# Placing VectorE's inversion of the softmax sums before or behind the row maximum in a fused attention and feed-forward kernel

## What is computed

```python
def _attn_ref(q, k, v) -> np.ndarray:
    B, H, S, D = q.shape
    factor = 2
    scale = 1.0 / np.sqrt(D)
    q_pool = q.reshape(B, H, S // factor, factor, D).mean(axis=3)
    scores = scale * np.matmul(q_pool, k.transpose(0, 1, 3, 2))
    scores = scores - np.max(scores, axis=-1, keepdims=True)
    attn = np.exp(scores)
    attn = attn / (np.sum(attn, axis=-1, keepdims=True) + 1e-09)
    return np.matmul(attn, v).astype(np.float32)
...
    h = x @ w_in
    g = np.maximum(h, 0.0) + alpha * np.minimum(h, 0.0)
    return (g @ w_out).astype(np.float32)
```

## Time and profile before

| | |
|---|---|
| median of 3 runs | 898.81 us (898.24 to 899.74) |
| the profiled execution | 899.53 us, span 897.7 us |
| TensorE matmul | 846.3 us, 94% of the span |
| TensorE weight load | 653.1 us, 73% (beside the matmuls) |
| VectorE | 517.0 us, 58% |
| ScalarE | 424.8 us, 47% |
| GpSimd | 406.7 us, 45% |
| granted TensorE clock, mean | 0.998 |
| attention | to about 480 us |

### The profile page before, as it was taken

The page is one execution under the profiler, slowest core; times in us unless marked ns, Lnnn a source line. Parts: engine busy times, 40 slices in busy tenths (PEclk is TensorE's granted clock), DMA queues, the critical chain, the costliest instruction groups (busy, mean ns, idle before and its releaser), DMA issues. The chain is left out here.

```text
span 897.7 us, 20876 instructions
## 1 busy us (share of the span) xinstructions
PE 846.3 (94%) x6897; PEld 653.1 (73%) x6897; DVE 517.0 (58%) x792; ACT 424.8 (47%) x939; POOL 406.7 (45%) x320
## 2 busy tenths in 40 slices
PE   2899999999999999999999999999999999999996
PEld 1566666666665656666566899998999998999995
DVE  3677677776777777777774443445444445444442
ACT  2566666666666666766663222224222224222222
POOL 3656557555575556755532223223323323332330
PEclk9999999999999999999999999999999999999999
DMA  7344454434544445434321221223222122312211
GB/s 166 110 121 101 122 144 123 119 94 121 143 124 99 111 125 143 114 99 106 84 81 62 60 70 58 61 67 99 90 60 69 58 71 85 104 58 68 61 36 70
DMA packets 37518, 84.37 MB, mean 94 GB/s; under 512 B 6512, under 2 KB 10608, under 8 KB 37488
## 3 DMA queue, kind: packets, MB, share of 16 engines
q1 hardware_dynamic: 35088, 79.27, 33.0%
q10 hardware_dynamic: 2400, 4.72, 1.5%
HBM read 79.18 MB, written 4.79 MB: 94 GB/s over the span
## 5 line engine op out<-in xcount | busy, mean ns | idle before, releaser
L769 PE MATMUL slot_ps<-kq 128*128 128x384 f32 x1152 | 218.0, 337 | 1.4 <-PEq L766 1.4
L769 PEld LDWEIGHTS slot_ps<-kq 128*128 128x128 f32 x1152 | 204.3, 188 | 11.2 <-issue 3.3
L550 DVE TENSOR_REDUCE neg_max<-s_ps 128x1 f32<-128x1152 f32 x144 | 194.8, 1353 | 20.6 <-DVEq L549 19.9
L785 PE MATMUL s_ps<-kq 128*128 128x512 f32 x720 | 182.4, 394 | 2.1 <-PEq L782 2.1
L690 PE MATMUL s_ps<-kq 64*128 64x512 f32 x960 | 151.5, 424 | 8.9 <-PEq L701 4.4
L453 ACT ACTIVATE e_sb<-s_ps,neg_max 128x1024 f32<-128x1024 f32 x144 | 159.8, 1110 | 0.0
L717 PE MATMUL pv_ps<-pt,v_f 128*64 128x256 f32 (+1 forms) x1152 | 155.1, 412 | 0.2 <-PEq L736 0.2
L785 PEld LDWEIGHTS s_ps<-kq 128*128 128x128 f32 x720 | 133.4, 188 | 26.6 <-issue 3.7
L405 POOL TENSOR_TENSOR kq<-wi_raw,kq 128x512 fp32r<-128x512 f32 x48 | 64.6, 1347 | 152.4 <-POOLq L404 152.4
L413 POOL TENSOR_TENSOR kq<-wo_raw,kq 128x512 fp32r<-128x512 f32 x48 | 64.5, 1343 | 139.6 <-POOLq L412 139.6
L717 PEld LDWEIGHTS pv_ps<-pt,v_f 128*64 128x64 f32 x1152 | 76.7, 136 | 68.7 <-issue 25.5
(11 more groups left out here) (49 smaller groups left out, 699.5 us busy)
## 6 DMA issues: line engine op xcount, KB each, us to landing
q_raw<-in_q SPq DMA_DIRECT2D x62, 320.0 KB, 4.3
k_raw<-in_k SPq DMA_DIRECT2D x62, 288.0 KB, 4.2
wi_raw<-in_w_in SPq DMA_DIRECT2D x48, 256.0 KB, 2.6
wo_raw<-in_w_out SPq DMA_DIRECT2D x48, 256.0 KB, 2.6
v_f<-in_v SPq DMA_DIRECT2D x32, 288.0 KB, 3.7
out<-pt ACTq DMA_DIRECT2D x6, 768.0 KB, 3.9
inv_bc<-sums SPq DMA_DIRECT2D x32, 80.0 KB, 2.6
inv_bc<-sums SPq DMA_DIRECT2D x32, 64.0 KB, 3.7
```

What stands on the lines that cost most here:

```text
L550: nc.vector.tensor_reduce(out=neg_max[:, b:b + 1], in_=s_ps[:, S_AT[b]:S_AT[b] + NKEY], op=ALU.max, axis=AX_X, negate=True).then_inc(max_r ...
L769: ins = nc.tensor.matmul(slot_ps[h][:, 0:TOK], w[i][:, d * P:(d + 1) * P], x[h][:, d * TOK:(d + 1) * TOK], start=(d == 0 and w is wi_hi an ...
L785: ins = nc.tensor.matmul(y_ps[h][t], g[h][:, t * P:(t + 1) * P], w[i], start=(first == 0 and j == 0), stop=(last == 1 and j == 2))
```

## The change

`INVERT` becomes two tables, one for each g, and the call moves from between the two copies to the end of VectorE's step, behind the row maximum. The inversion of group 1 that stood in steps t = 0 of g = 0 goes to t = 1. The last one, with no pair behind it, is called where `left` is negative, which is step 144 alone. The order on the other engines is unchanged, and the same instructions are issued.

```diff
--- before.py
+++ after.py
@@ -56,7 +56,9 @@
     PRODUCT = [{1: (1, 1, (0, 1, 2)), 3: (1, 1, (3, 4, 5)), 5: (1, 1, (6, 7, 8)), 7: (0, 0, (0, 1, 2, 3, 4))},
                {0: (0, 1, (5, 6, 7, 8)), 2: (1, 1, (0, 1, 2, 3, 4)), 4: (1, 1, (5, 6, 7, 8)),
                 6: (0, 0, (0, 1, 2, 3, 4)), 8: (0, 0, (5, 6, 7, 8))}]
-    INVERT = {5: 0, 0: 1}
+
+
+    INVERT = [{5: 0, 1: 1}, {5: 0, 0: 1}]
 
     SCALE = [{0: 0, 6: 1}, {1: 0, 5: 1}]
     FIRST = 7
@@ -583,8 +585,6 @@
                     dve.wait_ge(tr_ready[1], 1).then_inc(tr_ready[1], -1)
                     nc.vector.tensor_copy(pt_half((s - 1) % TILES, 1),
                                           half_columns(slot_ps[1][:, :])).then_inc(slot_free[1], 1)
-                if t in INVERT and (INVERT[t] == 0 or pair is not None):
-                    invert(INVERT[t])
                 if s % 2 == 0:
 
                     dve.wait_ge(bank2_ready, 1).then_inc(bank2_ready, -1)
@@ -595,6 +595,10 @@
 
                         dve.wait_ge(even_cut_done, 1).then_inc(even_cut_done, -1)
                     row_max(s + 2)
+                if t in INVERT[g] and (INVERT[g][t] == 0 or pair is not None):
+                    invert(INVERT[g][t])
+                elif left < 0:
+                    invert(1)
 
             def unit(f, h):
                 dve.wait_ge(h_ready, 1).then_inc(h_ready, -1)
```

## The result

The changed kernel takes 914.77 us (median of four runs, 911.15 to 916.04) against 899.27 for the kernel before (median of four): a ratio of 1.0167, 95% interval 1.0136 to 1.0198. The forecast was 903.9. The direction was right, the size was a third of what came. The profiled execution took 914.39, 14.9 more than that of before, and its span is 912.6.

The account below looks back on a forecast made before the run. TensorE, busy 94% of the span, was taken to bound the kernel. Seven repeats +2.2, the start +1.6 and the clock +1.3 sum to +5.1 on the median 898.81: 903.9 us, range 901.0 to 906.5.

Parts of the forecast that it names:

- The path: Inversion leaves the row maximum's chain and delays the next step's scale and `slot1` copy, so TensorE's pause moves.
- step 60 at +0.25: After the inversion of t = 5, g = 0: later scale and copy lengthen step 60 by 0.25 us.
- step 56 at -0.15: Group 1's inversion moved to t = 1, g = 0: row maximum comes sooner, step 56 0.15 us shorter.
- step 64 at +0.20: After the inversion of step 63: later scale and copy lengthen step 64 by 0.20 us.
- nothing lost at t = 5, g = 1 and at the end: Steps 14, 32, ... 140 and the last inversion (step 144): later inversions cost TensorE nothing, 0.
- no scale waiting for late sums after step 18: Later sums still reach their scale in time; the opposing rival, chance 0.06, gave 910.9.
- the chain at the start: Step 5's later store delays head 4's queries, GpSimd, head 5's keys and step 14's scale: +1.6 us.
- the fall of the clock behind it: Step 14's pause grows to about 3.5 us, the clock drops to half in steps 15 and 16: +1.3 us.
- The order terms: Seven repeats of 0.27, 0.20 and -0.15 us from the new order on VectorE: +2.2 us.
- t = 0, g = 1: Steps 27, 45, ... 135, shown for 63: inversion behind the row maximum delays scale and copy, +0.20 us each.
- The list of rivals: Five: clock stays up 902.6 (0.23); start hidden 901.0 (0.09); waits go 892.1 (0.07); nothing changes 898.8 (0.08); late sums 910.9 (0.06).
- The clock term: +1.3 us for half clock after step 14's pause; the rival that it stays up had 0.23, 902.6.

Follow-up runs that it names:

- the one-input run: Changed kernel with an inversion's two half-sums added by a reduction over one tensor, the 1e-9 left out; 905.79 us, ratio 1.0077.
- run 5: Kernel before with only the inversion of t = 5, g = 0 moved behind the row maximum in loop and tail, two inputs; 922.97 us, ratio 1.0255.
- run 4: Kernel before with only the inversion of t = 0, g = 1 moved behind the row maximum, two inputs; 911.16 us, ratio 1.0116.
- run 6: Kernel before with only the inversion of step 5 moved behind the row maximum; 904.28 us, ratio 1.0051.
- run 3: Changed kernel with the first inversion (step 5) back at its old place ahead of the row maximum; 908.84 us, ratio 1.0108.

## Why the prediction was wrong

**Right.** The path (pauses ahead of the ninth transposes turn into pauses ahead of the next step); step 60 at +0.25 and step 56 at -0.15, both within 0.01 in a repeat that meets no GpSimd; step 64 at +0.20, as the one-input run shows; nothing lost at t = 5, g = 1 and at the end, no scale waiting for late sums after step 18; the chain at the start and the fall of the clock behind it. The order terms sum to +2.2; the one-input run's repeat is 0.28 longer than that of before, seven times of which is 2.0.

**Wrong: the step "t = 0, g = 1".** It took for granted that the inversion has the same length wherever it stands ("its transpose starts 0.56 after the end of what is ahead of it"). The three instructions were costed from rows in which GpSimd was between two of its own. In the new place the sum takes 0.98 in six repeats and 1.96 in the seventh: +1.0 for each of six and +1.9 instead of +0.20, 7.9 instead of 1.4. The same sum, long in the inversions of steps 73, 109 and 127, delays the copy of the step behind and spoils the gain of 0.15 (step 74 takes 4.19, though step 76 gives 0.47 back); in those of steps 77 and 113 it makes the step behind, of step 60's kind, 4.3 to 4.4 long. Together these and the clock in step 137 are about 9 of the 15 us, which is what the one-input run gives back. The list of rivals had no such case. It would have needed one question for a moved instruction: what is every other engine doing at the new time, not only on the queues passed. GpSimd's timeline around 224 to 230 (run 5 shows its rows) has a subtraction from 226.48 to 229.13, just where the sum was to go: with the row maximum first the sum comes near 227.9, and 1.2 of the subtraction is left, or 1.0 once step 60 is 0.25 longer. Run 4 and the changed kernel show just that (1.22 to 1.28, and 0.98).

The Trainium skill ("SBUF — State Buffer", section "SBUF: two separate sides") states the rule: VectorE and GpSimd share one pair of ports to the on-chip memory as an exclusive lock, which is taken, among others, by a VectorE operation with two inputs there when GpSimd's operation reads there; whichever starts first has it for its whole instruction, and the other is blocked until then. The traces agree in each point that they can show: the sum with two inputs ends with GpSimd's instruction, the reduction with one never waits (0.157 at most), and the scale, one of whose inputs is in the accumulator banks, takes 0.49 at most throughout. The reverse is there too: a GpSimd subtraction that starts at 630.29, 0.55 us into a VectorE subtraction with two inputs there that takes 1.76, takes 2.37 instead of 1.30. By that rule the term would have been about 8 (an estimate, from the 1.0 above and the longer piece in step 135), and the forecast about 910.

**Mis-sized: the start.** Forecast 1.6 for the chain and 1.3 for the clock. Measured against step 5: GpSimd starts 3.4 later and step 15 3.1 later (36.66 instead of 33.53 after step 5), and the slow clock costs 1.9. Of the 1.8 missed in the chain to GpSimd 0.4 is a later row maximum in step 5, and about 1.2 a slower load of the queries behind the store (from its issue to GpSimd's start 6.7 instead of 5.5). In run 6, which moves the same inversion, that load took 5.4, so it does not follow from the move alone. What else the DMA engines carried then was not tried, so the cause of the slower load stays open.

The clock term was decided rightly, and the trace adds its price at both levels: the 20 products of step 15 take 3.78 here against 2.91 at full clock.

## What to carry to other kernels

An instruction's duration belongs to its place: before moving it, look at what the engine that shares its ports does at the new time, and prefer a form with one input in the on-chip memory (a reduction over a pair) to a sum of two tensors. Put small work that nobody waits for into the gap where its engine has nothing due, behind the last thing that the bottleneck needs, and look for such a gap in every step. A tuned order may rest on a gap of 0.18 us; a kernel that changes nothing in that place can still lose over 20 us there.

## What was not expected of the hardware

A VectorE sum of two 128x4 tensors, 0.15 us alone, took up to 2.59 us beside a GpSimd subtraction of 2.65 us that had started 0.08 earlier. The clock's fall to 1.2 GHz after short pauses of TensorE is not regular in one and the same kernel: in run 4 it fell after one of six pauses of 1.63 to 1.68 us, in run 5 after four of six of 2.81. In the changed kernel eight pauses of 1.37 to 1.61 passed without a fall, and those of 2.25 and 4.40 did not. In run 3 one of 2.23 passed without a fall and one of 1.65 did not.
